# Both heads of a pair scored side by side, and a new order of the attention steps inside the MLP's chunks

## The reference

```python
q_d, k_d, v_d = means of 4 neighbouring positions        # 144 positions
out_d = softmax(q_d k_d^T / 8) v_d, each row repeated 4 times
scores = q k^T / 8, kept where |i - j| < 4, else -1e9
x = out_d repeated + softmax(scores) v                   # float32
h = x @ w_in; x = (h * cos(h)) @ w_out                   # 512 -> 2048 -> 512
xn = x / rms(x) * g
y = (silu(xn @ w_gate) * (xn @ w_val)) @ w_out2          # 512 -> 1536 -> 512
```

## Time and profile before

| | us |
|---|---|
| median of 3 runs (971.92 to 973.64) | 973.09 |
| the profiled execution | 974.04 |
| its span, first to last instruction | 972.3 |
| TensorE matmuls busy | 951.9 |
| VectorE busy | 591.2 |
| ScalarE busy | 411.0 |
| GpSimd busy | 308.9 |
| loading a pair's queries and keys, issue to landing, median of 14 | 4.2 |

### The profile page before, as it was taken

How to read it: one execution, slowest core, us unless ns; L and a number is a source line. 1 busy time by engine, 2 the same in 40 slices (tenths; PEclk the granted TensorE clock), 3 DMA queues, 4 the chain that set the end, 5 groups by cost and what they waited for, 6 DMA issues and landing times.

```text
span 972.3 us, 17493 instructions
## 1 busy us (share of the span) xinstructions
PE 951.9 (98%) x6104; PEld 848.5 (87%) x6104; DVE 591.2 (61%) x1225; ACT 411.0 (42%) x889; POOL 308.9 (32%) x366
## 2 busy tenths in 40 slices
PE   7899999999999999999999999999999999999998
PEld 5678888888888899999989988899899899999997
DVE  6668777776876675675768554445644456544344
ACT  4435445544644454454544433334422234433232
POOL 5948873221422165486474220011200002000000
PEclk9999999999999999999999999999999999999999
DMA  9622211111111134354345665555565555575631
GB/s 290 219 71 99 79 54 54 54 53 54 53 55 53 50 128 150 130 195 169 140 161 185 261 210 148 152 157 159 146 217 151 152 161 162 154 227 162 163 98 65
DMA packets 66173, 132.31 MB, mean 136 GB/s; under 512 B 7088, under 2 KB 7216, under 8 KB 66096
## 3 DMA queue, kind: packets, MB, share of 16 engines
q1 hardware_dynamic: 66096, 131.27, 42.8%
HBM read 104.50 MB, written 26.74 MB: 135 GB/s over the span
## 4 chain that ended last, share of the span: by engine, by line
PE 91%; POOL 3%; DVE 2%; issue 1%; ACT 1%; DMA 1%; SPq 0%; POOLq 0%; ACTq 0%; DVEq 0%
PE ps L1268 28%; PE ps L1270 27%; PE ps L1269 27%; POOL W L519 2%; PE ps L1187 1%; PE ps L1204 1%; PE ps L1342 1%; PE ps L1245 1%; PE ps L1221 1%; PE ps L1237 1%; DMA qk<-qk 1%; PE ps L1224 1%; DVE xs L960 0%; POOL vg_more L493 0%; POOL prob L505 0%
## 5 line engine op out<-in xcount | busy, mean ns | idle before, releaser
L1268 PE MATMUL ps<-xo,wu 128*128 128x384 f32 x504 | 168.7, 335 | 1.5 <-DVE gate_a L1090 1.5
L1269 PE MATMUL ps<-xo,wu 128*128 128x384 f32 x504 | 169.9, 337 | 0.0
L1270 PE MATMUL ps<-xo,wu 128*128 128x384 f32 x504 | 169.4, 336 | 0.0
L1268 PE MATMUL ps<-xs,W 128*128 128x384 f32 x384 | 134.6, 350 | 0.9 <-DVE xs L960 0.9
L1270 PE MATMUL ps<-xs,W 128*128 128x384 f32 x384 | 130.5, 340 | 0.0
L1269 PE MATMUL ps<-xs,W 128*128 128x384 f32 x384 | 130.1, 339 | 0.0
L1268 PE MATMUL ps<-W,ring 128*128 128x512 f32 x288 | 116.4, 404 | 0.1
L1270 PE MATMUL ps<-W,ring 128*128 128x512 f32 x288 | 113.4, 394 | 0.0
L1269 PE MATMUL ps<-W,ring 128*128 128x512 f32 x288 | 113.2, 393 | 0.0
L751 ACT ACTIVATE ub<-ub,consts 128x384 f32<-128x384 f32 x96 | 59.1, 616 | 104.9 <-DVE ub L1049 104.2
L1268 PEld LDWEIGHTS ps<-xo,wu 128*128 128x128 f32 x504 | 94.7, 188 | 8.2 <-DVE gate_a L1090 1.8
(11 more groups left out here) (132 smaller groups left out, 1730.4 us busy)
## 6 DMA issues: line engine op xcount, KB each, us to landing
wu<-wsplit SPq DMA_DIRECT2D x252, 256.0 KB, 2.8
wsplit<-wp SPq DMA_DIRECT2D x84, 256.0 KB, 2.0
W_raw<-w SPq DMA_DIRECT2D x8, 1024.0 KB, 14.6
qk<-qk SPq DMA_DIRECT2D x14, 576.0 KB, 4.2
gv<-wgv SPq DMA_DIRECT2D x12, 512.0 KB, 3.7
vw<-vwin SPq DMA_DIRECT2D x14, 384.0 KB, 3.2
out<-XY SPq DMA_DIRECT2D x18, 256.0 KB, 3.6
vg<-vgrp SPq DMA_DIRECT2D x26, 144.0 KB
```

Of the source, the lines that this page charges most:

```text
L1268: t_.matmul(dst, a_lo, b_hi, start=first, stop=False, skip_group_check=True)
L1269: t_.matmul(dst, a_hi, b_lo, start=False, stop=False, skip_group_check=True)
L1270: return t_.matmul(dst, a_hi, b_hi, start=False, stop=last, skip_group_check=True)
```

## The change

The change touches only pairs in the chunks (`Narrow`). Both heads' steps now stand together: `local_both` sets the masks of both heads (head 0 in X, head 1 in Z) and issues the ten windows with the heads alternating; `downsampled_both` does the same with the downsampled scores, which now go where the local scores of the same head stood, and so waits until VectorE has read both (`diff_ready` 2n + 2). The two tables give way to three, one per engine, in which every pair has the same places counted from step 4j + 1. VectorE takes both differences, then both `down_max`, then each sum at a place of its own. `down_qk` stands two steps ahead of the pair's local scores. ScalarE's `exps` stand one step behind the local scores' step, and are ordered alike for both heads. The diff, without unchanged context and without the parts of VectorE's and TensorE's `attend` that only rename:

```diff
@@ -207,7 +207,7 @@
...
-        sl, sd = [X[:, 0:TP * WIN]] * 2, [Z[0:QT, 0:2 * SD]] * 2
+        sl, sd = [X[:, 0:TP * WIN], Z[:, 0:TP * WIN]], [X[0:QT, 0:2 * SD], Z[0:QT, 0:2 * SD]]
@@ -344,21 +344,15 @@
...
-    PE_STEPS = ("scores0", "local1", "downsampled1", "transposes0", "transposes1", "values")
-    PE_WHERE = (((1, 0), (2, 0), (3, 0), (4, 0), (4, 1), (5, 0)),
-                ((5, 1), (6, 0), (6, 1), (7, 1), (8, 0), (8, 1)),
-                ((9, 0), (9, 1), (10, 0), (11, 1), (12, 0), (12, 1)),
-                ((13, 0), (13, 1), (14, 0), (15, 0), (16, 0), (16, 1)))
-    BESIDE_STEPS = ("down_qk", "less_max0", "exps", "copy_pt0", "copy_pt1", "copy_down")
-    BESIDE_WHERE = (((-1, 1), (0, 0), (1, 1), (2, 1), (3, 1), (4, 1)),
-                    ((4, 0), (5, 1), (5, 1), (6, 1), (7, 1), (8, 1)),
-                    ((8, 0), (9, 0), (9, 1), (11, 0), (12, 0), (12, 1)),
-                    ((12, 0), (13, 0), (13, 1), (14, 1), (15, 1), (16, 1)))
+    PE_STEPS = ("local", "downsampled", "transposes0", "transposes1", "values")
+    PE_AT = ((0, 0), (1, 0), (2, 1), (3, 0), (3, 1))
+    DVE_STEPS = ("down_qk", "diff", "down_max", "sum0", "sum1", "copy_pt0", "copy_pt1", "add_up")
+    DVE_AT = ((-2, 1), (0, 0), (1, 0), (1, 1), (2, 0), (2, 1), (3, 0), (3, 1))
+    ACT_STEPS = ("exps", "copy_pt0", "copy_pt1", "copy_down")
+    ACT_AT = ((1, 1), (2, 1), (3, 0), (3, 1))
...
-        return [(name, j) for j in range(PAIRS) for name, at_ in zip(names, where[j]) if at_ == place]
+        return [(name, j) for j in range(PAIRS) for name, (step, half) in zip(names, where) if (4 * j + 1 + step, half) == place]
@@ -628,7 +622,7 @@
...
-            if kind is Narrow and s == 0:
+            if kind is Narrow:
@@ -965,21 +959,24 @@
...
-            for what, j in steps_at(BESIDE_STEPS, BESIDE_WHERE, (f, half)):
+            for what, j in steps_at(DVE_STEPS, DVE_AT, (f, half)):
...
-                elif what == "less_max0":
-                    less_max(Narrow, c + 1, j, 0)
-                elif what == "exps":
+                elif what == "diff":
+                    less_local_max(Narrow, c + 1, j, 0)
...
+                elif what == "down_max":
+                    down_max(Narrow, c + 1, j, 0)
+                    down_max(Narrow, c + 1, j, 1)
+                elif what == "sum0":
...
-                    down_max(Narrow, c + 1, j, 1)
+                elif what == "sum1":
...
-                elif what == "copy_down":
+                elif what == "add_up":
@@ -1163,50 +1160,66 @@
...
-        def local(kind, b, j, s):
-            n = PAIRS * b + j
-            u = 2 * n + s
-            q, k = (kind.qk[j][64 * s:64 * s + 64, a, :] for a in range(2))
-            if kind is Narrow:
-                if s == 0:
-                    pe.wait_ge(x_ready, n)
-                else:
-                    pe.wait_ge(diff_ready, u)
-            elif u > 1:
-                pe.wait_ge(diff_ready, u - 1)
-            if s == 0:
-                pe.wait_ge(kind.qk_in[j], 16 * loads(kind, b, j))
-            sl = kind.sl[s]
+        def masks(sl):
...
-            for w in range(NW):
-                half, t = w % 2, w // 2
-                ins = t_.matmul(sl[64 * half:64 * half + 64, t * WIN:t * WIN + WIN], q[:, Q0[w]:Q0[w] + WIN], k[:, K0[w]:K0[w] + WIN],
-                                start=False, stop=w >= NW - 2, skip_group_check=True)
-            ins.then_inc(local_scores, 1)
-        def downsampled(kind, b, j, s):
+        def local_window(kind, j, s, w):
+            q, k = (kind.qk[j][64 * s:64 * s + 64, a, :] for a in range(2))
+            half, t = w % 2, w // 2
+            return t_.matmul(kind.sl[s][64 * half:64 * half + 64, t * WIN:t * WIN + WIN], q[:, Q0[w]:Q0[w] + WIN], k[:, K0[w]:K0[w] + WIN],
+                             start=False, stop=w >= NW - 2, skip_group_check=True)
+        def downsampled_tile(kind, j, s, t):
+            q, k = (kind.qkd[j][64 * s:64 * s + 64, a, :] for a in range(2))
+            return t_.matmul(kind.sd[s][:, t * SD:t * SD + SD], q[:, t * QT:t * QT + QT], k, start=True, stop=True)
+        def scores(kind, b, j, s):
...
+            if u > 1:
+                pe.wait_ge(diff_ready, u - 1)
+            if s == 0:
+                pe.wait_ge(kind.qk_in[j], 16 * loads(kind, b, j))
+            masks(kind.sl[s])
+            for w in range(NW):
+                ins = local_window(kind, j, s, w)
+            ins.then_inc(local_scores, 1)
...
-            if kind is Narrow:
-                if s == 1:
-                    pe.wait_ge(exp_down, u)
-            elif u > 1:
+            if u > 1:
...
-            q, k = (kind.qkd[j][64 * s:64 * s + 64, a, :] for a in range(2))
...
-                ins = t_.matmul(kind.sd[s][:, t * SD:t * SD + SD], q[:, t * QT:t * QT + QT], k, start=True, stop=True)
+                ins = downsampled_tile(kind, j, s, t)
...
-        def scores(kind, b, j, s):
-            local(kind, b, j, s)
-            downsampled(kind, b, j, s)
+        def local_both(kind, b, j):
+            n = PAIRS * b + j
+            pe.wait_ge(x_ready, n)
+            pe.wait_ge(kind.qk_in[j], 16 * loads(kind, b, j))
+            for s in range(2):
+                masks(kind.sl[s])
+            for w in range(NW):
+                for s in range(2):
+                    ins = local_window(kind, j, s, w)
+            ins.then_inc(local_scores, 2)
+        def downsampled_both(kind, b, j):
+            n = PAIRS * b + j
+            pe.wait_ge(qkd_ready, n + 1)
+            pe.wait_ge(diff_ready, 2 * n + 2)
+            for t in range(2):
+                for s in range(2):
+                    ins = downsampled_tile(kind, j, s, t)
+            ins.then_inc(down_scores, 2)
```

More of the change, by code:

```diff
@@ L686, in attend @@
         def attend(c, f, half):
-            for what, j in steps_at(BESIDE_STEPS, BESIDE_WHERE, (f, half)):
+            for what, j in steps_at(ACT_STEPS, ACT_AT, (f, half)):
                 if what == "exps":
@@ L1291, in attend @@
         def attend(b, step, half):
-            for what, j in steps_at(PE_STEPS, PE_WHERE, (step, half)):
-                if what == "scores0":
-                    scores(Narrow, b, j, 0)
-                elif what == "local1":
-                    local(Narrow, b, j, 1)
-                elif what == "downsampled1":
-                    downsampled(Narrow, b, j, 1)
+            for what, j in steps_at(PE_STEPS, PE_AT, (step, half)):
+                if what == "local":
+                    local_both(Narrow, b, j)
+                elif what == "downsampled":
+                    downsampled_both(Narrow, b, j)
                 elif what == "transposes0":
```

## The result

The median of 12 runs is 978.02 us (974.75 to 979.92), against 972.31 for the kernel before (12 runs, 971.79 to 974.16). The ratio is 1.0049, 95% interval 1.0036 to 1.0061: the change makes the kernel **slower by 0.49%**, where I forecast no measurable change (972.9 us). 978.02 lies just past the upper end of my range. The profiled execution took 978.03 us with a span of 976.2; by the same account I had worked out 973.8, so 4.2 us are to be explained.

The account below looks back on a forecast made before the run. TensorE was taken to bound the kernel. 974.04 us, plus 7.3 for pair 0's waits, less 7.5 gained in pairs 1 to 3, gave 973.8 profiled; less 0.95, 972.9 us, no measurable change. Range 968.5 to 978.0.

Parts of the forecast that it names:

- the price of the scores: TensorE's scores per pair: 3.64 us before, 2.08 side by side (windows 1.24, downsampled 0.84), a gain of 1.56 us.
- The rival of serial windows: Neither the two heads' windows nor their downsampled scores run side by side: 0.58 us more in ten pairs, some 979 us; chance 0.05.
- the one of the start-to-start rule: Matmuls never start closer than about 25 ns, so 40 window passes need 1.0 us, not 0.6: 976.9 us; chance 0.01.
- Pair 0's downsampled scores: In chunks 1 and 2 TensorE stands there for VectorE's two differences, 160.18 to 162.35: 2.2 us.
- Its first transposes: Pair 0, chunks 1 and 2: probabilities ready at 170.33, TensorE wants them at 167.37 and waits 2.96 us.
- Pair 3's second transposes: Head 1's probabilities come 2.04 us after head 0's, TensorE is ready after 0.55: a wait of 1.5 us.
- The other first transposes: Pairs 1 to 3: probabilities ready at 7.34, TensorE wants them at 7.11, a wait of 0.23 us.
- The chain of 7.12 us: From VectorE's angle of step 2 (L1047) through exponentials and sums to TensorE's first transposes: 7.12 us.
- both rivals on its length: Chain to the transposes 0.3 us shorter: 969.9 us, chance 0.30; or 0.3 us longer: 976.5 us, chance 0.12.
- the clock falls: Pair 0's long waits in each chunk drop TensorE to 1.2 GHz, losing 1.6 us each time: 977.6 us; chance 0.09.
- hidden: Load of queries and keys for `down_qk`: median 4.2 us, issued 7 us ahead on VectorE, so it costs nothing.
- 18.7 us: TensorE's gain from cheaper scores over 12 pairs, nearly all of it expected to be stood away in waits.

Follow-up runs that it names:

- the first experiment: Only pair 3's steps moved forward on TensorE, VectorE and ScalarE, against the changed kernel: 973.95 us, ratio 1.0017 to the kernel before.

## Why the prediction failed

**Right: the price of the scores.** Windows alternating on both row halves: 1.13 us for the block against 1.24 less the 0.11 behind it, which I counted with it; 40 passes in 0.74 us. Downsampled scores: 0.64 for 8 passes, as the earlier trace rows had it for 4. The rival of serial windows fell with that, and the one of the start-to-start rule too: 0.74 us over 40 passes is 18.5 ns. The Trainium skill (TensorE: Matmul & The Clock Gate, "Wait — 56ns, not 53.3ns?") has matmuls never start closer than about 25 ns; this trace disagrees for passes on different parts of the array, since 40 of them would need 1.0 us.

**Right: each wait, and its size.** Pair 0's downsampled scores 2.14 us (worked out: 2.2). Its first transposes 17.67 us after the chunk's start (worked out: 152.66 to 170.33, also 17.67), a wait of 2.73 where the clock didn't shorten it (2.96). Pair 3's second transposes: from the first to the `down` behind them 2.72 us (236.97 to 239.69) where 0.55 and 0.6 are work, so a wait of 1.6 (1.5). The other first transposes: `down` and wait together 2.33 us instead of 2.09 (0.24, worked out 0.23). The chain of 7.12 us, eight links from eight rows of another pattern, held to a few hundredths, so both rivals on its length fell.

**Wrong: the clock's chance.** I had the mechanism, the place and the price among the rivals ("the clock falls", 1.6 us a time) and gave it 0.09; the sum had no term for it. It happened once in every chunk of the profiled execution and cost 3.2 us there; filling the waits took 3.1 us off by the ratios. The step that failed is "it decides if TensorE's wait in pair 0 is long enough for the gate, which no row of before shows". The kernel before had a granted clock of 1.00 in chunk 2 and, in its table of waits from 60 to 343 us, none above 0.5 us. That is no evidence that waits of 2 to 3 us are harmless. I also looked only at pair 0, and the fall in chunk 0 came behind pair 3.

Nor do show a fall behind an idle stretch, as I read them. The trace of before has the 20 passes of one head at its very start:

```profile
5.37 1.33 PE L1187 MATMUL ps<-qk 64*64 64x64 f32 x20
6.64 1.23 PE L1204 MATMUL ps<-qkd 64*72 64x144 f32 x4
```

They take 1.27 us from start to start, where they take 0.73 in the chunks, and no work ahead of 63.06 is faster than that. TensorE had been at 1.2 GHz from the start; what I took for a fall was the time before the first rise.

The section "HAM oscillation — how this bites in real kernels" of the same page of the Trainium skill describes the same kind of thing, waits that bring the clock down and are paid each time anew, and in kind the trace agrees, with three falls. The example of the Trainium skill in that section waits about 3 to 5 us each time; here no wait was above 2.8, and the clock fell all the same.

My own price for this rival was 977.6 us, 0.4 from what was measured. But that is partly luck: it counts three falls at full price, where one cost nothing, and has no late load.

**Wrong: "hidden".** For the load of queries and keys I set the median of 4.2 us against 7 us of room. Both were off in chunk 0, at pair 1. The load took 8.3 us, behind 1 MB of weights. And it isn't issued when the downsampled scores end (88.77 + 0.64 = 89.41) but at 91.50, because SP came to it only behind the three issues ahead of it in its program, and stood at the first of them, a load of value groups, until 90.26; that was 6.05 us before VectorE wanted it (97.55). The trace of before had this at the same place: issued at 92.87, behind W_raw at 91.22, it took 8.3 us there too, and nobody waited, since `down_qk` stood later. The median is taken over loads of which most have no such neighbour. And I named nothing behind `down_qk` that TensorE needs soon, though `copy_ptd` stands there. Cost: 1.3 us.

**The sum.** 973.8 + 3.2 + 1.3 = 978.3, against 978.03. The chunks leave +0.3 us beyond these terms, and chunk 0 began 0.66 us earlier than before, which is the execution and not the change: 978.3 + 0.3 - 0.7 = 977.9.

**Where the gain went**, then: of 18.7 us, the waits of pair 0 and pair 3 and the short ones at the others took all of it, and half clock and late load made a loss of 4 to 5 us. None of that is bound to the idea: with four placements mended and GpSimd's wait filled, the same side-by-side scores give 958.15 us. The edit on GpSimd wasn't run in the kernel before; with no wait of TensorE above 0.5 us there, I'd expect nothing from it.

**What stays open.** Which wait brings the clock down isn't settled. The wait of 2.54 us at pair 0 of chunk 0 (71.5 to 74.0) was followed by no fall in the profiled execution of the changed kernel. In five experiments with a wait of 1.9 to 2.6 us there, the clock fell between 73.8 and 75.6. So chance has a part in it, and what else has isn't shown.

The scatter is open too. The changed kernel runs from 974.75 to 979.92, the first experiment from 971.94 to 978.3, and its profiled execution is the lowest of them, so its trace isn't that of its median. Falls that cost 0 to 1.6 us, by their place, are one source. They aren't the only one: with the waits filled, nine of ten executions have a granted clock of 0.999 or 1.00 and still run from 972.61 to 975.88.

## What to carry to other kernels

When a change turns a full TensorE into one that waits 2 to 3 us several times, price the clock as the likely case, not as a tail: here each fall cost 1.6 us of work done behind it, and nothing if the stretch at half clock lay inside a wait. A transfer is hidden by its own row at that place, with what is queued ahead of it, not by the median of its kind. And when a cheaper block buys nothing, look at the waits one by one before giving it up: here they sat at three unrelated places, a fourth on GpSimd came to light behind them, and moving single steps by a place or two turned +0.5% into -1.6%.

## What the runs showed that I had not expected

- The kernel is faster with more work on TensorE. 84 matmuls without use, put into its waits, took 3.1 us off by the ratios (known to 1.6), and 1.6 us off the one chunk where nothing else differs, since the granted clock stayed at 1.00.
- What a fall costs depends on where it lies: 1.6 to 1.7 us when TensorE had work, nothing when it was waiting, between chunks with the same work and the same chain (96.01 and 94.33 us).
- How far passes of two heads on different row halves overlap depends on their order in the queue. 40 passes took 0.74 us with the heads alternating, 1.14 with 20 and then 20, and 1.46 would be no overlap; with 4 and then 4 (downsampled scores) the order made no difference, 0.64 and 0.65 us.
